# The own term of the dense stage's attention units: by token on GpSimd and VectorE, into the scores' diagonal, in place of key sums on TensorE

## The reference, cut to what matters

```python
def _attn_ref(r, k, v, w, u):                       # 4 batches, 8 heads, 768 tokens, head size 48
    state = np.zeros((B, H, D, D))
    for t in range(S):
        kt, vt, rt = (k[:, :, t], v[:, :, t], r[:, :, t])
        cur = np.einsum('bhd,bhe->bhde', u[None] * kt, vt)      # the own term
        y[:, :, t] = np.einsum('bhd,bhde->bhe', rt, state + cur)
        state = w[None, :, :, None] * state + np.einsum('bhd,bhe->bhde', kt, vt)
x = y as [3072, 384]
x = (silu(x @ w_gate) * (x @ w_val)) @ w_out        # dense stage, width 1536
e_idx = argmax(x @ gate); out = gate * sigmoid * (relu(x @ w1[e]) @ w2[e])   # 8 experts of width 1024
```

## Time and profile before

| | before |
|---|---|
| median of three runs | 846.97 us (846.66 to 848.94) |
| the profiled execution | 847.38 us |
| its span, first to last instruction | 845.4 us |
| TensorE busy | 830.3 us (98%) |
| VectorE busy | 474.1 us (56%) |
| ScalarE busy | 319.1 us (38%) |
| GpSimd busy | 177.7 us (21%) |
| mean granted clock of TensorE | 0.998 |

### The profile page before, as it was taken

How to read it: one execution, slowest core, us unless ns; L and a number is a source line. 1 busy time by engine, 2 the same in 40 slices (tenths; PEclk the granted TensorE clock), 3 DMA queues, 4 the chain that set the end, 5 groups by cost and what they waited for, 6 DMA issues and landing times.

```text
span 845.4 us, 20997 instructions
## 1 busy us (share of the span) xinstructions
PE 830.3 (98%) x8465; PEld 727.3 (86%) x8465; DVE 474.1 (56%) x1044; ACT 319.1 (38%) x523; POOL 177.7 (21%) x139
## 2 busy tenths in 40 slices
PE   6999999999999999999999999999999999999996
PEld 4778888788888887888778888899999999999996
DVE  7746444335533353435433444359979777887771
ACT  3523231113111131113111322357467666687661
POOL 3234013221423033303220210003120101111010
PEclk9999999999999999999999999999999999999999
DMA  8545112111221022302200105237996668776700
GB/s 321 185 141 170 58 32 86 59 60 39 94 83 59 6 92 63 114 1 75 86 18 2 39 20 193 89 157 246 346 391 251 241 245 326 271 258 244 288 18 20
DMA packets 24007, 115.89 MB, mean 137 GB/s; under 512 B 3356, under 2 KB 9680, under 8 KB 18304
## 3 DMA queue, kind: packets, MB, share of 16 engines
q1 hardware_dynamic: 19840, 100.24, 33.2%
q0 software_dynamic: 3520, 9.87, 3.1%
q10 hardware_dynamic: 576, 4.72, 1.6%
HBM read 101.73 MB, written 14.16 MB: 137 GB/s over the span
## 4 chain that ended last, share of the span: by engine, by line
PE 97%; DMA 1%; DVE 1%; issue 0%; ACT 0%; POOLq 0%; SPq 0%; DVEq 0%
PE bank L1679 35%; PE bank L1726 7%; PE bank L1727 6%; PE bank L1728 6%; PE bank L1799 5%; PE bank L1801 5%; PE bank L1800 5%; PE bank L1764 3%; PE bank L1766 3%; PE bank L1765 3%; PE bank L1760 3%; PE bank L1610 2%; PE bank L1596 1%; PE bank L1566 1%; PE bank L1519 1%; PE bank L1740 1%
## 5 line engine op out<-in xcount | busy, mean ns | idle before, releaser
L1265 DVE TENSOR_TENSOR PP<-SG,bank 128x512 f32<-128x512 f32 (+1 forms) x78 | 49.9, 647 | 234.6 <-PE bank L1679 171.8
L1679 PE MATMUL bank<-X1H,WH 128*128 128x512 f32 x432 | 168.5, 391 | 0.7 <-DVE X L1035 0.4
L1679 PE MATMUL bank<-X1L,WH 128*128 128x512 f32 x432 | 168.0, 390 | 0.2 <-DVE X1L L1088 0.2
L1679 PE MATMUL bank<-X1H,WL 128*128 128x512 f32 x432 | 168.0, 390 | 0.0
L823 ACT ACTIVATE SG<-bank 128x512 f32<-128x512 f32 x72 | 43.0, 597 | 235.4 <-PE bank L1679 235.4
L734 ACT ACTIVATE AH<-PP 128x512 fp32r<-128x512 f32 (+1 forms) x78 | 46.1, 598 | 160.4 <-DVE PP L1265 160.4
L1679 PEld LDWEIGHTS bank<-X1H,WH 128*128 128x128 f32 x432 | 81.0, 188 | 18.3 <-issue 1.3
L1679 PEld LDWEIGHTS bank<-X1H,WL 128*128 128x128 f32 x432 | 81.0, 188 | 17.3 <-DVE WL L1082 0.3
L1679 PEld LDWEIGHTS bank<-X1L,WH 128*128 128x128 f32 x432 | 81.0, 188 | 17.0 <-DVE X1L L1088 0.7
L1726 PE MATMUL bank<-AH,WH 128*128 128x512 f32 (+1 forms) x234 | 92.2, 394 | 0.0
L1728 PE MATMUL bank<-AH,WL 128*128 128x512 f32 (+1 forms) x234 | 87.6, 374 | 0.0
(11 more groups left out here) (238 smaller groups left out, 1773.8 us busy)
## 6 DMA issues: line engine op xcount, KB each, us to landing
W_EVEN<-w SPq DMA_DIRECT2D x20, 1536.0 KB, 8.5
W_ODD<-w SPq DMA_DIRECT2D x18, 1536.0 KB, 7.6
RK_IN<-unit_rk SPq DMA_DIRECT2D x19, 736.0 KB, 5.4
V_IN<-unit_v SPq DMA_DIRECT2D x20, 448.0 KB, 3.4
STG<-w_dense ACTq DMA_DIRECT2D x4, 1152.0 KB, 5.3
XG_ODD<-store SPq DMA_DIRECT2D x9, 394.0 KB, 8.0
store<-PAD SPq DMA_DIRECT2D x8, 394.0 KB, 5.0
STG<-w_dense SPq DMA_DIRECT2D x2, 1152.0 KB, 9.2
```

The source lines that it names most:

```text
L1265: return tt(PP[:, part], SG[:, part], VALUE_PS[:, part], ALU.mult)
L1679: last = mm(bank_[:, :], lhs[:, f, m, k * P:k * P + P], rhs[:, k, :], start=(x == 0), stop=(x == len(terms) - 1))
```

## The change

Key sums, RXK and `own_key` go from the 20 units of the dense stage. In their place: R by token (`rt`) comes with V in place of V by column; GpSimd multiplies it with K by token (`own_products`) and with u (`weight_own`, in place in OWN); VectorE sums over the 48 (`sum_own`, two reductions); ScalarE makes eight 64x64 diagonal blocks by scaling a unit matrix with those sums (`diagonals`, to DIAG); VectorE adds them to `AM` after masking (`add_diagonals`), which alone now releases `outputs`. For that `AM` gets four blocks of 64 tokens for each pair (zeros, swapped head's diagonal, other head's diagonal, rest), and the scores' bank three. In an odd step ScalarE copies the first bank of the outputs to X1 (`copy_output`) and VectorE adds only the second. The first chunk's units keep the old way. TensorE's waits for the gate sums, for `c_used` and for the silu ahead of the unit are taken out.

```diff
-    AM_PARTS = AM[:, :].rearrange("p (x q t) -> p x q t", x=2, q=2)
-    ZEROS, SHORT, LONG = slice(0, P // 2), slice(P // 2, P), slice(P, 2 * P)
+    AM_PARTS = AM[:, :].rearrange("p (x q b t) -> p x q b t", x=2, q=2, b=4)
+    AM_DIAG = AM[:, :].rearrange("p (xq c) -> p xq c", xq=4)[:, :, P // 2:P // 2 + P]
+    own_factors = OWN[:, 0:PAIRS * PR]
...
-            sp.dma_start(causal, consts[:, C_CAUSAL:C_ALL]).then_inc(causal_loaded, 16)
+            sp.dma_start(CST[:, C_CAUSAL:C_ALL], consts[:, C_CAUSAL:C_ALL]).then_inc(causal_loaded, 16)
+            sp.dma_start(BONUS[:, :], consts[:, C_BONUS:C_DRAM]).then_inc(bonus_loaded, 16)
             sp.dma_start(WROUTE[:, :, :], w_route).then_inc(route_loaded, 16)
...
+            def own_products(u):
+                u.wait_rk(pool)
+                u.wait_v(pool)
+                need(pool, own_summed, u.i - BATCH)
+                nc.gpsimd.tensor_tensor(own_factors, u.rk[:, I_KT:I_RK], u.v[:, I_RT:I_VR], ALU.mult).then_inc(own_made, 1)
+
+            def weight_own(u):
+                pool.wait_ge(own_made, u.i - BATCH + 1)
+                nc.gpsimd.tensor_tensor(own_factors, own_factors, BONUS[:, :], ALU.mult).then_inc(own_weighted, 1)
...
             def scale_without_kt(u):
-                scale_rk(u)
+                own_products(u)
                 scale_k(u)
+                weight_own(u)
                 scale_r(u)
 
             def scale_units(n):
@@ -678,13 +701,16 @@
             scale_rk(u2)
             scale_rk(u3)
             u4 = units_of_block(0)[0]
-            scale_rk(u4)
+            u4.wait_rk(pool)
             scale_r(u4)
             pool.wait_ge(keys_turned, BATCH - 1)
             scale_k(u4)
             pool.wait_ge(dense_low, 3)
+            pool.wait_ge(keys_loaded, 16)
+            own_products(u4)
+            pool.wait_ge(bonus_loaded, 16)
+            weight_own(u4)
             pool.wait_ge(tables_ready, 1)
-            pool.wait_ge(keys_loaded, 16)
             scale_kt(u4)
             scale_units(0)
...
+
+            def diagonals(u):
+                act.wait_ge(causal_loaded, 16)
+                act.wait_ge(own_summed, u.i - BATCH + 1)
+                act.wait_ge(masked, 2 * u.i)
+                for two in HEADS_OF_PAIRS:
+                    for a in two:
+                        last = nc.scalar.activation(DIAG[:, a.x, a.pair, a.short_block, :], unit64, ACT.Copy,
+                                                    scale=OWN_SUM[:, a.x, a.s:a.s + 1])
+                last.then_inc(diag_made, 1)
+
+            def copy_output(u, n):
+                act.wait_ge(x1_low, KT * n + KT)
+                act.wait_ge(y_ready, u.i + 1)
+                copy(X1[:, :, u.out], u.y[0][:, 0:DM].rearrange("p (k t) -> p k t", k=KT)).then_inc(half_added, 1)
 
             def x1_high_part(b):
...
+                    if f // 2 < len(units):
+                        if f % 2 == 0:
+                            diagonals(units[f // 2])
+                        else:
+                            copy_output(units[f // 2], n)
...
                         made = u.scores[half][:, :].rearrange("p (j t) -> p j t", j=PAIRS)
-                        last = tt(u.am[:, half, :, :], made, mask.unsqueeze(1).broadcast_to([P, PAIRS, P]), ALU.mult)
+                        tt(u.am[:, half, :, :], made, mask.unsqueeze(1).broadcast_to([P, PAIRS, P]), ALU.mult).then_inc(masked, 1)
                     else:
                         made = u.scores[half][:, 0:2 * PART].rearrange("p (q t) -> p q t", q=2)
-                        last = tt(u.am[:, half, :, SHORT.start:LONG.stop], made, causal.unsqueeze(1).broadcast_to([P, 2, PART]), ALU.mult)
-                    last.then_inc(masked, 1)
+                        to = u.am[:, half, :, 1:4, :].rearrange("p q b t -> p q (b t)")
+                        tt(to, made, causal.unsqueeze(1).broadcast_to([P, 2, PART]), ALU.mult).then_inc(parts_masked, 1)
...
+            def sum_own(u):
+                dve.wait_ge(own_weighted, u.i - BATCH + 1)
+                need(dve, diag_made, u.i - BATCH)
+                for x in range(2):
+                    last = nc.vector.tensor_reduce(OWN_SUM[:, x, :], own_factors.rearrange("p (s c) -> p s c", s=PAIRS)[:, :, 64 * x:64 * x + HD],
+                                                   AX.X, ALU.add)
+                last.then_inc(own_summed, 1)
+
+            def add_diagonals(u):
+                dve.wait_ge(diag_made, u.i - BATCH + 1)
+                dve.wait_ge(parts_masked, 2 * u.i - 2 * BATCH + 2)
+                tt(AM_DIAG, AM_DIAG, DIAG[:, :, :, :, :].rearrange("p x q b t -> p (x q) (b t)"), ALU.add).then_inc(masked, 2)
 
             def add_output(u):
-                dve.wait_ge(c_used, u.i + 1)
                 dve.wait_ge(y_ready, u.i + 1)
-                last_of_y = u.y
-                if not u.first:
-                    first_of_y, last_of_y = u.y
-                    tt(X1[:, :, u.out], first_of_y[:, 0:DM].rearrange("p (k t) -> p k t", k=KT), X1[:, :, u.out], ALU.add)                        .then_inc(half_added, 1)
+                if u.first:
+                    dve.wait_ge(c_used, u.i + 1)
+                    y = u.y
+                else:
                     dve.wait_ge(half_added, u.i - BATCH + 1)
-                last = tt(X1[:, :, u.out], last_of_y[:, 0:DM].rearrange("p (k t) -> p k t", k=KT), X1[:, :, u.out], ALU.add)
+                    y = u.y[1]
+                last = tt(X1[:, :, u.out], y[:, 0:DM].rearrange("p (k t) -> p k t", k=KT), X1[:, :, u.out], ALU.add)
                 last.then_inc(y_added, 1)
```

```diff
@@ dense_block of VectorE @@
-                            own_key(u)
+                            sum_own(u)
                             mask_scores(u)
...
+                            add_diagonals(u)
@@ TensorE @@
-            def key_sums(u):
...
         def scores_in_parts(u):
...
+                        to = u.scores[a.x][a.long, a.pair * PART:(a.pair + 1) * PART].rearrange("p (b t) -> p b t", b=3)
+                        mm(to[:, a.long_blocks, :], u.kw[a.rows, a.keys][:, EARLIER],
+                           u.rw[a.rows, a.keys].rearrange("p (b t) -> p b t", b=2), start=True, stop=True)
...
         def outputs(u):
...
+                            blocks = slice(a.long_blocks.start + 1, a.long_blocks.stop + 1, a.long_blocks.step)
+                            mm(u.y[a.long is LATER][p.out, p.cols].rearrange("p (b t) -> p b t", b=2),
+                               u.v[a.long, a.v:a.v + VW][:, p.cut], u.am[a.long, a.x, a.pair, blocks, :],
...
         def state_terms(u):
-                    pe.wait_ge(c_used, u.i + 1)
...
         def dense_block(n):
-                    if f % 2 == 1 and f // 2 < len(units):
-                        pe.wait_ge(gate_sums_used, units[f // 2].i + 1 - BATCH)
...
-                            pe.wait_ge(silu_ready, q + 1)
...
-                            key_sums(u)
```

More of the change, by code:

```diff
@@ L61 @@
 PART = P + P // 2
-C_ALL = C_CAUSAL + PART
+C_UNIT = C_CAUSAL + PART
+C_ALL = C_UNIT + P // 2
+C_BONUS = C_ALL
+C_DRAM = C_BONUS + PAIRS * PR
 STRIP = 32
@@ L86, in __init__ @@
         self.pair = self.s // 2
+        self.long_blocks, self.short_block = (slice(0, 3, 2), 0) if self.swapped else (slice(1, 3), 1)
         self.used = slice((VW - HD) * (h % 2), (VW - HD) * (h % 2) + HD)
@@ L192, in rwkv_moe_moe @@
     RK_IN = [place(a, f"RK_IN{b}", [P, I_RK]) for b in range(2)]
-    V_IN = [place(a, f"V_IN{b}", [P, I_VV]) for b in range(2)]
+    V_IN = [place(a, f"V_IN{b}", [P, I_VR]) for b in range(2)]
     KW = place(a, "KW", [PR, PAIRS * P])
-    RXK = place(a, "RXK", [PR, PAIRS * P])
+    OWN = place(a, "OWN", [P, PAIRS * P])
+    BONUS = place(a, "BONUS", [P, PAIRS * PR])
+    OWN_SUM = place(a, "OWN_SUM", [P, 2, PAIRS])
+    DIAG = place(a, "DIAG", [P, 2, 2, 2, P // 2])
     RW = place(a, "RW", [PR, PAIRS * P])
@@ L813, in dense_block @@
                 last = isinstance(n, int) and n == CH - 1
+                units = [] if last else units_of_block(n)
                 if not first:
@@ L1511, in _ @@
         def _(pe):
-            def key_sums(u):
-                pe.wait_ge(rxk_scaled, u.i + 1)
-                pe.wait_ge(c_used, u.i)
-                pe.nop(nofuse=True)
-                opened = set()
-                for p in BOTH:
-                    a, at = p.head, (p.head.x, p.out.start)
-                    last = mm(u.c_banks[a.x][p.out, p.cols], SELU[a.rows, a.s, p.cut], u.rxk[a.rows, a.keys],
-                              start=at not in opened, stop=True, skip_group_check=True)
-                    opened.add(at)
-                last.then_inc(c_ready, 1)
             def first_key_sums(ua, ub, second):
@@ L1609, in outputs @@
                             a = p.head
[L1610 to L1611 removed]
+                            blocks = slice(a.long_blocks.start + 1, a.long_blocks.stop + 1, a.long_blocks.step)
+                            mm(u.y[a.long is LATER][p.out, p.cols].rearrange("p (b t) -> p b t", b=2),
```

(10 more changed lines are left out.)

70 lines of the change are left out of this document (34 added, 36 removed).

## The result

The changed kernel takes **837.97 us**, median of 4 runs (836.86 to 838.4), against 847.25 for the kernel before beside it (846.66 to 848.94): a ratio of 0.9885, interval 0.9868 to 0.9903. That is 9.3 us off, where 11.7 were forecast. The profiled execution took 837.9, with a span of 836.1 against 845.4. So the direction held, the time lies inside the range of 833 to 840.5, and 2.4 us of the forecast gain are missing. The rest of this document is mostly about those.

What follows compares the result with a forecast made beforehand. TensorE, busy 98% of the span, was taken as the bound. Gains of 11.9 and 0.4 less a loss of 0.6 gave 11.7 us off, forecast 835.5 us, range 833 to 840.5.

Steps and rivals of the forecast that it cites:

- Part 1: Dense stage, 20 units: dropping the key sums on TensorE saves 11.9 us, plus 0.4 from a vanished gate wait.
- Rival A: At the key sums, a drain stays or small matmuls only hide something: 9 us or less saved, 838 to 839; chance 0.08.
- Part 2: TensorE's scores and outputs matmuls with operands two blocks apart cost 0; the other end was 10 us in all.
- Rival C: Two-block operands in TensorE's matmuls count as two, up to 10 us: 846, no change; chance 0.05.
- Part 3: Each slot's own-term chain of sums, copies and diagonal addition ends before outputs, slack 2.0 us; cost 0.
- Rival D: Diagonals late for outputs in each of 20 slots, with all three terms 3.3 us late: 861; chance 0.04.
- Part 4: First block: new work delays the weight splits, so WL is late for the gate of f=2; loss 0.6 us.
- over 2 us ahead: First block: splits of weight pieces after f=2 are ready over 2 us before their gates; no loss put there.
- Rival B: First block costs 3 or 4 us, ScalarE's splits pushed further in each even step: 838 to 840; chance 0.08.

Runs made afterwards that it cites:

- Experiment 1: Changed kernel with the own term left out in its 20 units (no products, sums, copies or additions): 834.87 us, ratio 0.9852.
- experiment 6: Changed kernel with ScalarE's eight diagonal copies made twice from the second block on, first into a spare tile: 852.18 us.
- Experiments 2: Changed kernel with R by token loaded behind K instead of behind V, so GpSimd's products do not wait for V: 835.51 us, ratio 0.9863.
- experiment 8: Changed kernel with GpSimd's products of units 6, 7 and 8 held until the step's WL subtractions are done: 836.2 us, ratio 0.9871.
- Experiments 7: Changed kernel with R by token loaded with the keys, and the first unit's sums ahead of AL in step 0: 835.83 us, ratio 0.9871.
- 9: Changed kernel with GpSimd's products of units 6 to 8 held behind the WL subtractions and the first unit's sums before AL: 835.41 us, ratio 0.9865.
- experiment 10: Changed kernel with products of units 6 to 8 and unit 5's weighting held behind WL subtractions, first sums before AL: 834.7 us, ratio 0.9854.
- experiment 3: Changed kernel with only four of the eight diagonal copies made in the first block by the units after the first: 836.77 us.

## Why the prediction was right, and where its sum was off

- **Part 1, the key sums: right.** The steps in the trace are 0.59 to 0.60 in 19 slots and 0.47 plus 0.45 (the gate's vanished wait included) in the first. Experiment 1 gives 12.4 for what was put at 12.3. Rival A is out: the distance of starts was the right measure, not the union of 13.3, and no drain stayed behind.
- **Part 2, operands in two blocks: right at 0.** The groups agree to 0.1 us with those before. Rival C is out.
- **Part 3, the slot's chain: right.** The reductions took 0.60 for two where 0.72 was estimated, the copies 2.02 where 1.74 was taken, the addition 0.77 for 0.7; slack 1.7 for 2.0. The first slot of the second block has 1.5 (addition ended 127.06, outputs 128.55) for 1.8. The row taken for the copies was the nearest form but read PSUM, with 112 partitions, and these read SBUF with 128; this kernel's traces do not say which of the two makes the 0.28. The Trainium skill ("ScalarE: Activation LUTs", What ACT_TABLE_LOAD costs) has the terms for an ACTIVATE from which the forecast estimated 1.9; the last of eight has nothing to overlap with, so they come to an estimate of 2.0, and the trace agrees with 2.02. Rival D did not come, though experiment 6 shows that lateness there is dear: 1.94 us of extra copies turn a gain of 9.3 into a loss of 5.1.
- **Part 4, the first block: the step that failed.** "Loss 0.1 to 1.0, I take 0.6", and behind it "Splits of later pieces stand over 2 us ahead of their gate." The gate of f=2 was within reach: the lows were ready at 41.1 and TensorE lost 0.84 there, 1.0 with its slower restart. Those 1.0 are the top of its "0.1 to 1.0". But f=4, 6 and 8 cost 0.97, 0.52 and 0.31 and their restarts 0.4 more, 2.2 in all, where nothing had been put. Together that is 3.2 by the starts, and 3.1 by experiment 1: in place of 0.6.
- **Why that step failed.** The prediction shows no working for "over 2 us ahead", but the rows show what it takes: with subtractions of 2.68 the lows of f=4 would be ready at 51.94 + 2.68 = 54.62, and TensorE would come to that gate at 56.87 (57.84 less the 0.97 lost), 2.2 later. They took 5.84 and ended at 57.78. The prediction had the sign that they would not stay at 2.68: 3.62 beside GpSimd, 2.68 without, and rival D's argument that "two such instructions exclude each other". That was applied to the slot's addition, where there was slack, and to the lows of f=2, and not to the later lows, where two multiplications replaced one and waited for V. Experiments 2 and 8 give the collision as the cause of the three later waits; either one removes them, 2.2 and 2.4 us of the 3.1. At the first wait, at f=2, both the later split and the collision have a part. Experiments 7 and 9 (earlier split, worse collision) win 0.3 of it, and experiment 10 (earlier split, no collision) wins all. By the rows the collision alone would account for it: 37.32 + 2.70 = 40.02, against a gate that TensorE would have reached at 40.33 (41.17 less 0.84). That is worked out and not run.
- **Rival B** gave 838 to 840 by a first block that costs 3 or 4 us, and the time is 837.97 with 3.1 lost there. Its place and its size were nearer than the forecast's. Its mechanism is not what decided: the splits are pushed by 3.6 to 4.2 us in three even steps, as it said, but experiment 8 keeps that delay and loses nothing at f=4, 6 and 8. That the time still fell inside the stated range is owed to the width left for A, B and C, and not to a reading of these collisions.
- **The lock as the skill tells it.** The subtractions take 5.84 beside GpSimd's multiplications and 2.69 without. Two inputs from SBUF on VectorE against an SBUF reader on GpSimd is what the Trainium skill ("SBUF — State Buffer", Who interferes with whom) names, and the trace agrees. The forecast weighed that rule in rival D and left it out for the lows of f=4, 6 and 8, where it decided.

The missing 2.4 us are then the 2.5 of that one term (3.1 less 0.6), less the 0.1 by which Part 1 came out better.

## What to carry to other kernels

Before a change gives GpSimd an instruction or VectorE one with two SBUF inputs, list what else of that kind runs in the same stretch, in the one-time phases as well as in the steady slot; a collision in a warm-up block costs time too, once it is longer than the cover there. Cover such as "over 2 us ahead" has to be worked out with the price that the covered work will have among its new neighbours, here 5.84 and not 2.68. Where such a collision is the cause, a wait that holds GpSimd back until VectorE's stretch is over can be a cheap remedy: here it gave back 2.4 of the 3.1 us, and with a second hold and the early sums all of it, with GpSimd idle enough to pay for it.

## What the runs showed that was not expected

- **A small shift changes who pays.** With GpSimd's product ahead of VectorE's addition by 0.28 to 0.92 us (changed kernel), the two engines took turns, and three subtractions that take 2.69 alone took 5.84. In experiment 3, with VectorE 0.3 ahead, or behind by 0.06 and 0.11, four of its instructions ran back to back and GpSimd's single product took 3.99 to 4.41. 1 us less work on ScalarE was enough to change one into the other. What sets the order when they meet that closely is not shown.
- **A wait costs TensorE more than the view shows.** The four waits sum to 2.0, and the lead lost there is 3.2. Half of the rest is how the view counts: it begins a wait at the end of the matmul before, 0.39 after its start (40.11 to 40.50 at f=2), while undisturbed ones start 0.23 apart, so each of the four leaves out 0.16. The other half comes after the wait: the first two matmuls start 0.33 to 0.34 apart, and the gate is 0.12 to 0.17 longer. In experiment 6 the waits of the AM addition and the lows are 12.6 more than in the changed kernel (11.9 and 0.7), and the stretch from the state terms to the end is 14.3 longer.
- **ScalarE's copies hide as long as the chain has slack.** ScalarE is 49 us busier than before, and with GpSimd held none of that shows in the time. Eight copies more for each of 16 units use up the slack and cost 14 (experiment 6).
